# Second MLP: another order of VectorE's and ScalarE's work around the turn between its two stages, and S2 sums one step ahead of their splits

## The reference

```python
def _moe2_ref(x, w_in, w_out):      # x 4608 x 512, w_in 512 x 2048, w_out 2048 x 512
    h = x @ w_in
    g = np.where(h >= 1.0, h, np.where(h <= -1.0, 0.0, (h + 1.0) ** 2 / 4.0))
    return (g @ w_out).astype(np.float32)
```

## Time and profile before

| | |
|---|---|
| median of 3 runs | 1794.07 us (1793.14 to 1794.13) |
| the profiled execution | 1794.17 us, its span 1791.8 us |
| TensorE busy | 1734.6 us (97%), 9216 matmuls |
| TensorE's weight loads busy | 1541.4 us (86%) |
| VectorE busy | 839.2 us (47%) |
| ScalarE busy | 717.5 us (40%) |
| GpSimd busy | 314.2 us (18%), none of it after the first 1000 us |
| granted TensorE clock | 1.000 |
| moved by DMA | 300.48 MB |

### The profile page before, as it was taken

The page is one execution under the profiler, slowest core; times in us unless marked ns, Lnnn a source line. Parts: engine busy times, 40 slices in busy tenths (PEclk is TensorE's granted clock), DMA queues, the critical chain, the costliest instruction groups (busy, mean ns, idle before and its releaser), DMA issues. The chain is left out here.

```text
span 1791.8 us, 24808 instructions
## 1 busy us (share of the span) xinstructions
PE 1734.6 (97%) x9216; PEld 1541.4 (86%) x9216; DVE 839.2 (47%) x1220; ACT 717.5 (40%) x1033; POOL 314.2 (18%) x654
## 2 busy tenths in 40 slices
PE   7999999999999999999999998998999999989988
PEld 6888888888888888888888897998998988989988
DVE  3332323323233232332322366767677568568565
ACT  2332323323233232332321265565565565555553
POOL 5731414415144151441100000000000000000000
PEclk9999999999999999999999999999999999999999
DMA  5423414324143341433201276786776777877764
GB/s 214 156 77 99 138 55 154 104 98 143 48 155 104 106 139 43 154 107 105 78 24 59 94 267 234 241 301 225 258 283 234 259 269 243 283 258 244 246 236 169
DMA packets 97937, 300.48 MB, mean 168 GB/s; under 512 B 9760, under 2 KB 53792, under 8 KB 80928
## 3 DMA queue, kind: packets, MB, share of 16 engines
q1 hardware_dynamic: 87456, 251.69, 40.6%
q10 hardware_dynamic: 10368, 47.19, 7.8%
HBM read 250.61 MB, written 48.23 MB: 167 GB/s over the span
## 5 line engine op out<-in xcount | busy, mean ns | idle before, releaser
L1033 DVE TENSOR_TENSOR g_full<-val_ps,act_buf 128x512 f32<-128x512 f32 x108 | 74.7, 692 | 475.3 <-PE val_ps L514 446.7
L622 PE MATMUL banks<-split_hi,ring 128*128 128x384 f32 x672 | 228.1, 339 | 25.4 <-DVE split_lo L1153 25.0
L599 PE MATMUL banks<-combo_hi,ring 128*128 128x384 f32 x672 | 228.3, 340 | 18.7 <-ACT chain L830 18.7
L624 PE MATMUL banks<-split_hi,ring 128*128 128x384 f32 x672 | 225.0, 335 | 0.0
L623 PE MATMUL banks<-split_lo,ring 128*128 128x384 f32 x672 | 224.8, 335 | 0.0
L601 PE MATMUL banks<-combo_hi,ring 128*128 128x384 f32 x672 | 224.8, 335 | 0.0
L600 PE MATMUL banks<-combo_lo,ring 128*128 128x384 f32 x672 | 224.8, 334 | 0.0
L783 ACT ACTIVATE g_hi<-g_full 128x512 fp32r<-128x512 f32 x108 | 68.2, 631 | 287.5 <-DVE g_full L1033 287.5
L512 PE MATMUL gate_ps<-x_hi,weights 128*128 128x512 f32 x432 | 175.7, 407 | 0.1
L543 PE MATMUL out_ps<-g_hi,weights 128*128 128x512 f32 x432 | 171.6, 397 | 0.0
L545 PE MATMUL out_ps<-g_hi,weights 128*128 128x512 f32 x432 | 168.8, 391 | 0.0
(11 more groups left out here) (112 smaller groups left out, 3031.3 us busy)
## 6 DMA issues: line engine op xcount, KB each, us to landing
ring<-w_out_split SPq DMA_DIRECT2D x84, 1024.0 KB, 5.0
ring<-w_in_split SPq DMA_DIRECT2D x48, 1024.0 KB, 5.2
ring<-w_in_split SPq DMA_DIRECT2D x48, 768.0 KB, 6.6
tile_in<-q_k_dram ACTq DMA_DIRECT2D x33, 768.0 KB, 4.7
tile_in<-v_dram ACTq DMA_DIRECT2D x33, 512.0 KB, 3.8
w_in_split<-stage SPq DMA_DIRECT2D x112, 128.0 KB, 1.7
w_out_split<-stage SPq DMA_DIRECT2D x112, 128.0 KB, 1.8
x_in<-x_scratch SPq DMA_DIRECT2D x6, 1536.0 KB, 9.2
```

Of the source, the lines that this page charges most:

```text
L599: pe.matmul(ps, w_lo, hi, start=first and k == 0, stop=False, skip_group_check=more)
L622: pe.matmul(ps[:, j, :], w_lo, hi, start=first and k == 0, stop=False, skip_group_check=more)
L624: last = pe.matmul(ps[:, j, :], w_hi, hi, start=False, stop=k == NU - 1, skip_group_check=more)
```

## The change

On VectorE, in unit m, `add22(m-1)` moves ahead of `act12(m-2)`, and the split of units 5 to 7 moves from the end of a unit to the place behind the next `add22`: splits 0 and 1 into units 6 and 7, split 2 behind the loop. Behind the loop `act21(7)` moves ahead of split 3, `act12(7)` from behind splits 6 and 7 and the first S2 sum to a place between split 6 and that sum, and the S2 sums are each made one step earlier. On ScalarE `relu21(7)` moves ahead of split 3 and split 4 ahead of `relu12(7)`. No instruction is added or taken away, and TensorE's and SyncE's orders stay.

```diff
@@ ScalarE @@
                 relu1(p, NU - 1)
                 square1(p, NU - 1)
+                relu21(p, NU - 1)
                 split_part(p, KP - 1)
-                relu21(p, NU - 1)
+                split_part(p, KP)
                 relu12(p, NU - 1)
-                for s in range(KP, SPLITS):
+                for s in range(KP + 1, SPLITS):
                     split_part(p, s)
@@ VectorE @@
                 for m in range(1, NU):
+                    add22(p, m - 1)
+                    if m > NU - KP + 1:
+                        split_part(p, m - 1 - (NU - KP + 1))
                     if m >= 2:
                         act12(p, m - 2)
-                    add22(p, m - 1)
                     if m in (3, 5, 7):
                         tile_sums(p, (m - 3) // 2)
                     act21(p, m - 1)
                     max1(p, m - 1)
                     add12(p, m - 1)
                     add11(p, m)
-                    if m >= NU - KP + 1:
-                        split_part(p, m - (NU - KP + 1))
+                add22(p, NU - 1)
+                split_part(p, KP - 2)
                 act12(p, NU - 2)
-                add22(p, NU - 1)
                 max1(p, NU - 1)
+                act21(p, NU - 1)
                 split_part(p, KP - 1)
                 add12(p, NU - 1)
                 split_part(p, KP)
-                act21(p, NU - 1)
+                tile_sums(p, KP - 1)
                 split_part(p, KP + 1)
-                tile_sums(p, KP - 1)
                 split_part(p, KP + 2)
+                act12(p, NU - 1)
+                s2_sum(p, 0)
                 split_part(p, KP + 3)
-                s2_sum(p, 0)
-                act12(p, NU - 1)
+                s2_sum(p, 1)
                 for s in range(2 * KP, SPLITS):
                     split_part(p, s)
-                    if s < 3 * KP - 1:
-                        s2_sum(p, s + 1 - 2 * KP)
+                    if s < 3 * KP - 2:
+                        s2_sum(p, s + 2 - 2 * KP)
```

## The result

The changed kernel takes 1732.38 us (median of 4 runs, 1730.24 to 1734.57) against 1793.83 (4 runs, 1793.14 to 1794.13): a ratio of 0.9658, 95% interval 0.9641 to 0.9675. Five more executions gave 0.9668 (0.9655 to 0.9682). The forecast was 1736.2 in a range of 1734.5 to 1746; the measured median lies 2.1 us under the range.

The account below looks back on a forecast made before the run. The prediction took TensorE's waits on VectorE's splits and ScalarE's chain copies, 9.85 us a pass, as the bound. Less 0.2 left, six passes save 57.9: 1794.1 - 57.9 = 1736.2 us, range 1734.5 to 1746.

Parts of the forecast that it names:

- What bounds the kernel: Second MLP: TensorE's waits in four places take 9.85 us a pass, 59.1 us over six passes.
- Part 1: Product loop: add22 first, split after it, cuts the round under 7.28 us; waits of 1.49 and 2.12 go.
- Part 2: Turn from unit 7 to the output products: earlier add22(7) and split 3 shrink a 3.00 us wait to about 0.15.
- the residue: Waits left at two tight splits, split 3 and split 5: 0.1 to 0.2 us a pass plus another 0.05.
- Part 3: Later output pairs, after split 3: S2 sums one step ahead stop the 2.79 us alternation; 3.24 us a pass goes.
- 1794.1 - 57.9: Whole kernel: old time less six passes of 9.65 us saved gives 1736.2 us.
- (a): Rival: the turn keeps a real wait of 0.5 to 1.7 us a pass, 1738 to 1745 us; chance 0.16.
- (b): Rival: only the product loop improves, the turn stays bound; 4 to 6 us a pass stay, 1759 to 1771; chance 0.04.
- (c): Rival: transfers become the bound, needing 280 GB/s; a pass could stay 126.3 us, 1794 in all; chance 0.02.
- (d): Rival: slower, a circle at the turn makes act21(7) late, by 10.4 us or more to decide; chance 0.02.
- (e): Rival: no change, because another engine's queue holds the same round; chance 0.01.
- The weighed rule: VectorE operations start only once the pipe has emptied: 0.08 us per free neighbour, 0.55 a pass, near 1740; chance 0.01.

Follow-up runs that it names:

- experiment 2: Only the product loop in the new order, everything behind the loop as before the change: 1768.27 us, ratio to before 0.9856.
- experiment 3: Old product-loop order with split 2 at its end, all behind the loop and on ScalarE as in the changed kernel: 1766.46 us, ratio to before 0.9856.
- Experiment 9: The changed kernel with one extra 128x128 operation on VectorE in unit 7, ahead of max1(6): 1735.55 us, a pass of 116.69.
- experiment 4: The changed kernel with the S2 sums one step later, as before the change: 1742.55 us, a pass of 117.92.

## Why the prediction was right, and where it was wrong

- **What bounds the kernel** held: 9.85 us a pass of waits, six passes. A pass fell by 9.83, and the second MLP by 58.9 us against the 59.1 counted.
- **Part 1**, the loop's round cut from 9.40 and 7.40 to under 7.28 us, held; experiment 2 shows it alone, experiment 3 its absence.
- **Part 2**, the turn, held in its chain: split 3 starts at +14.49 for +14.51. One step that failed is the size of the residue, "I count 0.1 to 0.2 a pass" at o1.3, with "another 0.05" for split 5: it measured nothing that a trace can tell, 116.50 us a pass against 116.48 of slots, just under the 116.6 to 116.9 that I had named as the sign of being right. Split 3 ended at +15.44, 0.03 before my count, and "too little for its weight load to run ahead" was wrong: the load ran 0.11 us ahead, which was just enough. Experiment 9 shows how near that is to the edge: 0.2 later costs 0.19. Without the residue, 1.2 us in all, the sum gives 1735.0, a bound that I had worked out and that the range took in. This step alone would not have put the result outside it.
- **Part 3** held in its outcome: experiment 4 puts 1.42 us a pass on the sums' place. But of the 3.24 that it explains mostly by the sums, only 1.8 were lost at o6.1 to o6.3; 1.3 were lost at o5.0 and o5.2, which the prediction does not take up by themselves. They go with the new order of the turn (experiment 3 has neither, experiment 2 still waits 0.57 us at o5.0 of its first pass). For act12(7) alone there is no experiment.
- **What I had no term for** is the start, and this is the step that put the result outside the range. "1794.1 - 57.9" takes all that lies outside the waits as fixed; its runs known beforehand lay within 1 us. Two of the changed kernel's four runs lie on the lower level, which in the five kernels profiled there went with the clock up some 10 us sooner (20 us against 30 to 32), and the median fell between the levels, at 1732.4, where the two upper runs lie at 1734.3 and 1734.6. No choice of the terms that I had reaches under 1735.0, so the range had 0.5 us for a start that varies by 4. Of the miss of 3.8 us, 1.2 are the residue, 2.1 the levels, and 0.5 a spread that I can't put down to anything. The two levels are shown; what decides between them is not.
- **The rivals.** (a) did not come, but only just: 0.2 us more work costs 0.19 a pass (experiment 9). (b) is experiment 2, built on purpose; it came out at 1768, inside its 1759 to 1771. (c) is refuted: the pass moves 280 GB/s. (d) and (e) did not occur.
- **The weighed rule.** The operations behind splits 1 and 2 of after start 0.88 later for a length of 0.96, as before. The sum by the rule, near 1740, is not what came. The section of the Trainium skill that the prediction cites ("VectorE: DVE Perf Modes", "The DRAIN you can't avoid") goes on to say that a next operation starts earlier when it is not held (made to wait for those in front of it), and the prediction left that out; the 0.88 is in line with it.

## What to carry to other kernels

Where two engines hand work to each other in a round, add up the round from one start to the next and compare it with what the bounding engine needs; an operation that waits for the latest result of the round goes first in its queue, and those with slack (here act12 and the split) behind it. Two parts of such a change may only pay in full together (4.05 and 4.20 apart, 9.83 together). When waits can be removed altogether, weigh the case of none left as a case of its own, and do not take a few runs that agree for all that the start of a kernel can do. When a matmul seems to have a little to spare, look at its weight load, which needs the operand first.

## What the runs showed of the hardware

A split that ends 0.16 us before its matmul starts is only just in time: the weight load starts 0.05 us behind the split, and 0.20 us more work cost 0.19 us a pass, with a wait of 0.24 written at the load and none at the matmul.

And the clock can fall within the second MLP too. Experiment 2 waits 2.33 to 2.39 us at o1.3 of each of its six passes. In three of them, passes 2 to 4, TensorE then runs for about 3 us at the 1.2 GHz level; in the other three it does not, nor in any pass of the kernel before, which waits 2.40 to 2.50 us at the same place. Pass 2, in windows (length, TensorE busy, granted clock, DMA share, GB/s):

```profile
1214.00:1218.90 4.90, 2.53 (x15) 0.98 0.68 234
1218.90:1222.00 3.10, 3.08 (x10) 0.50 0.74 312
1222.00:1226.00 4.00, 4.00 (x24) 0.98 0.56 178
```

That pass was no longer than the others (122.28 us): passes 1 and 5, at the full clock, wait another 0.57 us at o5.0, where pass 2 has no wait. Why the same wait lowers the clock in one pass and not in the next is open. In the profile after, which has no such wait, the clock is 1.00 over the whole of pass 2.
